# Decay attention, expert layer and gated convolution in one kernel: the start-up order of the constants, the zeros and the first loads

## The reference, cut to what matters

```python
# 1. attention with a per-head decay lam, no softmax; out per block of the sequence:
intra = (q @ k.T) * Dmask          # Dmask[i, j] = lam ** (i - j) where i >= j, else 0
out   = intra @ v + (q * lam ** (pos + 1)) @ kv_state
kv_state = lam ** block * kv_state + (k * lam ** (block - 1 - pos)).T @ v
# 2. mixture of 8 experts; each token goes to one expert e (its own argmax, or the token before's)
out = softmax(logits)[e] * (relu(x @ w1[e]) @ w2[e])
# 3. depthwise convolution of 5 taps, sigmoid, times x @ w_val, then @ w_out
```

## Time and profile before

| | |
|---|---|
| time, median of 3 runs | 390.23 us (389.72, 390.23, 396.63) |
| the profiled execution | 392.58 us, span from first to last instruction 390.7 us |
| PE busy | 374.4 us (96%) |
| DVE / ACT / POOL busy | 239.2 / 178.1 / 106.0 us |
| mean granted TensorE clock | 0.978 of full speed |
| DMA | 70.10 MB, 179 GB/s over the span |

### The profile page before, as it was taken

The page is one execution under the profiler, slowest core; times in us unless marked ns, Lnnn a source line. Parts: engine busy times, 40 slices in busy tenths (PEclk is TensorE's granted clock), DMA queues, the critical chain, the costliest instruction groups (busy, mean ns, idle before and its releaser), DMA issues.

```text
span 390.7 us, 6744 instructions
## 1 busy us (share of the span) xinstructions
PE 374.4 (96%) x2528; PEld 346.0 (89%) x2528; DVE 239.2 (61%) x488; ACT 178.1 (46%) x305; POOL 106.0 (27%) x98
## 2 busy tenths in 40 slices
PE   7999999999899999999999999999997989969987
PEld 7999999998898999989899898989996978959876
DVE  7656786687657192664728357283721799892930
ACT  1133354332126363645628355463711774937352
POOL 5325688484100000000000000000006865352640
PEclk9989999899999999999999999999999889998999
DMA  7999968341614739475692947645014601002012
GB/s 236 418 412 399 398 192 308 121 161 55 213 58 173 259 123 351 152 257 193 217 320 107 323 138 277 228 161 216 2 53 137 192 1 54 29 0 81 3 54 107
DMA packets 30761, 70.10 MB, mean 179 GB/s; under 512 B 2320, under 2 KB 2832, under 8 KB 30224
## 3 DMA queue, kind: packets, MB, share of 16 engines
q1 hardware_dynamic: 26192, 59.25, 42.4%
q0 software_dynamic: 1920, 6.29, 4.9%
q10 hardware_dynamic: 2624, 4.22, 2.9%
HBM read 55.08 MB, written 14.68 MB: 179 GB/s over the span
## 4 chain that ended last, share of the span: by engine, by line
PE 79%; DVE 12%; issue 3%; DMA 2%; ACT 2%; POOL 1%; DVEq 0%; POOLq 0%; ACTq 0%
PE bank L1161 75%; DVE gate L1109 5%; DVE w_raw L1109 3%; PE bank L1215 2%; PE bank L1316 2%; DVE x_all L1082 1%; DMA x_all<-y_slots,gather_u 1%; DMA lam_all<-lam 1%; DVE decay L846 1%; DMA y_slots<-y_out 1%; PE bank L1391 1%; POOL x_all L521 0%; ACT gate L751 0%; DVE w_sp L1074 0%; ACT w_sp L716 0%
## 5 line engine op out<-in xcount | busy, mean ns | idle before, releaser
L1161 PE MATMUL bank<-w_sp,h_sp 128*128 128x512 f32 (+1 forms) x480 | 106.4, 380 | 0.0
L1161 PEld LDWEIGHTS bank<-w_sp,h_sp 128*128 128x128 f32 x480 | 86.4, 188 | 16.3
L1161 PEld LDWEIGHTS bank<-x_sp,w_sp 128*128 128x128 f32 x768 | 93.2, 192 | 0.9 <-issue 0.3
L1161 PE MATMUL bank<-x_sp,w_sp 128*128 128x256 f32 x768 | 93.8, 283 | 0.1
L949 DVE TENSOR_TENSOR w_sp<-w_raw,w_sp 128x1024 fp32r<-128x1024 f32 x60 | 70.8, 1221 | 12.3 <-ACT w_sp L596 12.1
L596 ACT ACTIVATE w_sp<-w_raw 128x1024 fp32r<-128x1024 f32 x68 | 68.6, 1057 | 13.6 <-PE bank L1161 13.6
L521 POOL DMA_INDIRECT x_all<-y_slots,gather_u x12 | 12.4, 1030 | 193.0 <-DMA y_slots<-y_out 189.7
L1026 DVE SCALAR_TENSOR_TENSOR h_sp<-bank,h_sp 128x512 fp32r<-128x512 f32 x32 | 22.1, 689 | 63.6 <-ACT h_sp L636 62.6
L1161 PE MATMUL bank<-w_sp 128*128 128x384 f32 x192 | 39.1, 361 | 3.9 <-DVE prod L1124 1.7
L1161 PEld LDWEIGHTS bank<-w_sp 128*128 128x128 f32 x192 | 36.2, 204 | 6.1 <-DVE w_sp L1074 2.8
L636 ACT ACTIVATE h_sp<-bank 128x512 fp32r<-128x512 f32 x32 | 19.1, 598 | 48.1 <-PE bank L1161 48.1
(11 more groups left out here) (131 smaller groups left out, 443.5 us busy)
## 6 DMA issues: line engine op xcount, KB each, us to landing
w_raw<-w SPq DMA_DIRECT2D x32, 1024.0 KB, 5.8
qkv_sb<-qkv SPq DMA_DIRECT2D x22, 512.0 KB, 9.6
x_slots<-zeros SPq DMA_DIRECT2D x4, 1024.0 KB, 14.2
x_in<-x_slots SPq DMA_DIRECT2D x7, 512.0 KB, 6.6
y_slots<-y_out ACTq DMA_DIRECT2D x7, 512.0 KB, 5.3
out<-x_in SPq DMA_DIRECT2D x11, 256.0 KB, 2.0
w_raw<-w_val SPq DMA_DIRECT2D x1, 1024.0 KB
w_raw<-w_out SPq DMA_DIRECT2D x1, 1024.0 KB
```

What stands on the lines that cost most here:

```text
L1161: return nc.tensor.matmul(o, lhsT, rhs, start=start, stop=stop, skip_group_check=free)
```

## The change

SP issues tiles 2 and 3 straight behind tiles 0 and 1, then waits for `zeros_ok` alone, and then issues the four writes of zeros. POOL no longer clears `zeros`; DVE does, after its small tables and `hold`, and waits for that itself. DVE then waits for `lam_all` and runs the 8 decay scans and `k_decay`, which now releases `decay_ok`. The constants for the routing and `lam_pair` become `route_constants()`, called behind `mask(0)` and ahead of the `q_decay` scans. PE's first warm-up is 8 products, not 12.

```diff
@@ sync
             load_tile(0)
             load_tile(1)
+            load_tile(2)
+            load_tile(3)
             sp.wait_ge(zeros_ok, 1)
-            sp.wait_ge(warm_ok, 1)
             for n in range(SLOTS * DM // (P * UNIT)):
...
-                if n < 2:
-                    load_tile(2 + n)
@@ gpsimd
-            nc.gpsimd.memset(zeros[:, 2 * P:UNIT], 0.0).then_inc(zeros_ok, 1)
             pool.wait_ge(decay_ok, 1)
@@ vector
-            link(nc.vector.memset(no_add[:, :], 0.0))
+            nc.vector.memset(no_add[:, :], 0.0)
+            nc.vector.memset(hold[:, :, :], 0.0)
+            nc.vector.memset(zeros[:, 2 * P:UNIT], 0.0).then_inc(zeros_ok, 1)
+            dve.wait_ge(zeros_ok, 1)
             dve.wait_ge(lam_in, 16)
-            for s in range(2):
-                r = slice(s * D, (s + 1) * D)
-                last = nc.vector.tensor_copy(lam_pair[r, :], lam_all[r, :].rearrange("p (a s) -> p s a", s=2)[:, s, :])
-            link(last)
             dve.wait_ge(ident_ok, 2)
             for h in range(H):
...
-            dve.wait_ge(consts_ok, 5)
...
-            link(nc.vector.tensor_copy(k_decay[:, :, :], decay[:, :, :, P - 1:P].rearrange("p s a o -> p a (s o)")))
-            nc.vector.memset(hold[:, :, :], 0.0).then_inc(decay_ok, 1)
+            nc.vector.tensor_copy(k_decay[:, :, :],
+                                  decay[:, :, :, P - 1:P].rearrange("p s a o -> p a (s o)")).then_inc(decay_ok, 1)
+
+            def route_constants():
+
+                dve.wait_ge(consts_ok, 5)
...
+                for s in range(2):
+                    r = slice(s * D, (s + 1) * D)
+                    last = nc.vector.tensor_copy(lam_pair[r, :], lam_all[r, :].rearrange("p (a s) -> p s a", s=2)[:, s, :])
+                link(last)
...
                 mask(t)
                 if t == 0:
+                    route_constants()
@@ tensor
             pe.wait_ge(warm_ok, 1)
-            warm(12, ps_route)
+            warm(8, ps_route)
```

More of the change, by code:

```diff
@@ L848, in _ @@
             link(last)
-            dve.wait_ge(consts_ok, 5)
[L850 to L855, removed]
-            link(nc.vector.tensor_copy(k_decay[:, :, :], decay[:, :, :, P - 1:P].rearrange("p s a o -> p a (s o)")))
-            nc.vector.memset(hold[:, :, :], 0.0).then_inc(decay_ok, 1)
+            nc.vector.tensor_copy(k_decay[:, :, :],
+                                  decay[:, :, :, P - 1:P].rearrange("p s a o -> p a (s o)")).then_inc(decay_ok, 1)
+            def route_constants():
+                dve.wait_ge(consts_ok, 5)
+                nc.vector.tensor_copy(iota8_ps, iota8[:, :])
+                nc.vector.memset(ones_ps, 1.0)
+                nc.vector.memset(fresh_below[0:1, :], ALWAYS_FRESH)
+                nc.vector.tensor_copy(route_rhs[0:E, 0:E], ident[0:E, 0:E])
+                nc.vector.tensor_copy(route_rhs[0:E, E:E + 1], iota_col[:, :])
+                nc.vector.memset(route_rhs[Q:Q + E, E + 1:E + 2], 1.0)
+                for s in range(2):
+                    r = slice(s * D, (s + 1) * D)
+                    last = nc.vector.tensor_copy(lam_pair[r, :], lam_all[r, :].rearrange("p (a s) -> p s a", s=2)[:, s, :])
+                link(last)
             def mask(t):
```

## The result

The changed kernel takes 393.52 us (median of 14 runs), the kernel before 390.67 us in its 14 runs beside them. The ratio is 1.0079 with an interval of 1.0046 to 1.0111, so the change costs 3.1 us (1.8 to 4.3). That is less than the 2% that count here as a difference, and more than I forecast: 390.7 with a range up to 393.2, against 393.5. The changed start, as the traces show it, explains only part of the 3.1 us, so a second cause has to be found.

The account below looks back on a forecast made before the run. PE, busy 96% of the span, was taken as the bound, with time to save only at the start. From 390.23 us, -1.0 for the decay chain and +1.5 for the clock gave 390.7 us, range 388.0 to 393.2.

Parts of the forecast that it names:

- the sum: Whole kernel: -1.0 us for the decay chain, +1.5 for the clock, 0 for the rest, +0.5 in all.
- The behaviour behind 10 us is shifted as a whole: Everything after the start: moves with the start's change, with no further cost of its own.
- the clock's: PE at the start: the idle gap after the shorter warm-up brings a low clock over the scores, costing 1.5 us.
- one stretch of 3.4 us: PE from 6.6 to about 10 us: low clock over the scores, price taken as 1.6 us before deducting 0.1.
- the bound of 3.3: PE at the start: highest price of the low clock, 3.3 us, if it lasts until about 13.4 us.
- the likeliest case: Start: earlier decays gain 1.0 us, low clock over the scores costs 1.5; median 390.7 us, chance 0.47.
- rival (b): PE at the start: low clock outlasts the scores; if until 13.4 us, loss 2.3, 392.5 us; chance 0.10.
- rival (a): PE at the start: clock is high at the scores and stays high, only -1.0 stands, 389.2 us; chance 0.33.
- The clearing: DVE at the start: clearing the zeros takes 1.55 us, bounds 1.5 to 1.9, ending at 3.4 us.
- the gain: PE's keys_values(0): moves from 10.07 to 9.1 us through earlier decays, gain 1.0 us, bounds 0 and 1.1.
- Rival (c): Start: tile 0's second half lands near 8.8 us or decay_ok comes no earlier; say 391.2 us; chance 0.10.
- The constants: DVE behind mask(0): nine small routing instructions and lam_pair, 0.6 and about 0.4 us, cost 0 to 0.3, taken as 0.

Follow-up runs that it names:

- old_loads: The changed kernel with tiles 2 and 3 issued between the zero writes again, as before the change; ratio 1.0047 to the kernel before.
- again: The changed kernel itself, unaltered, run once more for a second profile; ratio 1.0079 to the kernel before.
- pad4: The changed kernel with 4 warm-up products more at the end of the attention stage, restoring PE's instruction count; ratio 1.0009 to the kernel before.
- warm4: The changed kernel with 4 products in the first warm-up instead of 8; ratio 1.0036 to the kernel before.
- late6: The changed kernel with 6 first warm-up products instead of 8, begun only when DVE has cleared the zeros; ratio 0.9992 to the kernel before, 0.9974 when repeated.
- late8: The changed kernel with its 8 warm-up products begun only when POOL has cleared the state; ratio 0.9980 to the kernel before.
- before_warm8: The kernel before with 8 first warm-up products instead of 12, nothing else; no ratio, six runs from 394.57 to 418.30 us.
- lam_act: The changed kernel with lam_all issued on ScalarE's queue, 11 first warm-up products and one more at the attention stage's end; ratio 0.9984 to the kernel before.

## Why the prediction was wrong

**The step that failed** is the last sentence of the sum: "The behaviour behind 10 us is shifted as a whole". A transfer 290 us later did not shift: it grew. The warm-up's four products were priced for the gap that they leave and not for their eight records of code. Their absence moved a 16 KB piece of program in among the data packets of the one write that all else waits for. That term was put at nothing; it measured 1.3 us up to the first gather in the shown pair of profiles, up to 1.7 in the others, 1.9 (to some 1.3) at the end of the spans, and 0.8 (to 1.4) by the timings. None of the rivals had it.

**A term of the right kind and too small** is the clock's. Forecast at 1.5, it is 1.8 in the traces and 2.4 (to 1.4) by the timings. The gap was 1.83 us (2.12 in the first profile; forecast 1.85), and a low stretch came in every trace with a gap. Its price can be added up from the same four groups of PE, against their full rate (1.68, 0.71, 1.13, 1.90). In the first profile of after it is 0.71 + 0.51 + 0.35 + 0 = 1.6; in old_loads 0 + 0.47 + 0.84 + 0.36 = 1.7: about the 1.6 taken for one stretch of 3.4 us, though it began later than thought. In `again` it is 1.38 + 0.51 + 0.78 + 0.12 = 2.8 and in pad4 3.2, nearly the bound of 3.3 that stood for a stretch to 13.4. On the first transposes these four are 0.33, 0.37, 1.59 and 1.84 later than in the kernel before, a mean of 1.0, where the forecast had a net 0.5. By price, the likeliest case and rival (b), in which the low clock outlasts the scores and which was given 0.10, came twice each (and (b) once more in warm4); in old_loads the scores themselves were fast, as rival (a) had it, and the low stretch came behind them. With 1.0 for the start and about 1.5 for the write the sum is 2.5, inside the measured 1.8 to 4.3.

**What held.** The clearing took 1.55 us; the scans ended at 6.45 (forecast 6.1; the clearing started 0.3 late); `k_scaled(0)` was then held by the second half of tile 0, at 8.11 (forecast 7.9, landing 8.0 rather than 7.8), so most of DVE's gain of 2.1 us was lost to that transfer, as said. With the clock left alone the gain was 0.8 (forecast 1.0). Rival (c) thus didn't come. POOL in fact did nothing while the 8 scans ran, and they took the 2.63 us of the earlier trace rows.

**What POOL beside the scans would have cost** is shown by the four scans of `q_decay`, which have two SBUF inputs as well. In the kernel before they took 2.15 us beside this:
```profile
10.50 1.23 POOL L463 TENSOR_TENSOR k_scaled<-qkv_sb,k_decay 128x512 f32<-128x512 f32 x1 [0.58 <-DMA qkv_sb<-qkv]
```
In the kernel after, with POOL idle by then:
```profile
12.24 1.37 DVE L961 TENSOR_TENSOR_SCAN q_decay<-lam_pair,no_add 128x128 f32<-128x128 f32 x4
```
In all traces it is 1.37 without POOL (five) and 2.15 to 2.25 beside `k_scaled` (eight). That agrees with the sharing that the Trainium skill describes, and the order of the change does well to keep POOL out of the way of the first scans.

**What cost nothing.** The zeros were issued from 5.7 us and the last landed at 7.3 + 19.6 = 26.9, ahead of the scatter. The second halves of tiles 2 and 3 landed 9.1 and 10.6 after their issues, by 15.6, and nobody was waiting. The constants, eight small instructions and not nine, took 1.7 us, from 10.49 to 12.2 (forecast 1.0), and delayed no one on the chain, which stays on PE.

**The range** ended at 393.2 because it reached to the dearest case of the start and to no further cause; the time lies 0.3 beyond. That it lies outside is partly chance: the forecast counted from 390.23, the median of three runs, and with 14 runs the kernel before has 390.67, 0.4 more. What is off without that chance is the size of the change, 3.1 (1.8 to 4.3) against 0.5.

**What stays open.** How the 3.1 us divide between the two causes in the timed runs is known only to about 1.4 us. Why PE is at the low level behind the gap for about 3 us in one execution and 6 in another isn't known, nor why the packet of program takes 1.0 us in one and 1.6 in another.

Lastly, late6 and late8 beat the changed kernel (0.9974 to 0.9992 against 1.0079; the intervals are apart, that of late6 by 0.0004 only), but not clearly the kernel before. What is left to win at the start, 0.7 us, is below what these timings tell.

## What to carry to other kernels

A warm-up belongs right in front of the work it is for. If it is shortened, shorten it at its beginning, by a wait in front of it, and leave no gap behind it: the same eight products ended in first transposes at 16.64 or at 14.30. When the number of instructions of an engine changes, read again the transfers that everything waits for, however far behind they are, for their landing and for an "instruction" queue among their packets; put the count back with work that waits anyway to see whether that is the cause. And when an engine is taken off the path, look for the transfer behind it first: of 2.1 us on DVE, 0.8 were there to be had.

## What the runs showed of the hardware

- Behind an idle gap of 1.6 to 2.1 us that followed 3.4 to 4.3 us of work, PE came to stand at its 1.2 GHz level in all six traces that have one (seven with warm4 and its 3.45 us). In `again`, pad4 and warm4 it was at the low rate already in the warm-up and stayed there to about 13 us. In the first profile of after, in old_loads, before_warm8 and lam_act it had risen, fell at 7.5 to 8.5, and stayed low for about 3 us in the first two and 14 in the others. In the kernel before, 1.10 us of idle time behind the scores cost nothing.
- The granted clock shows 1.00 ahead of its first record in a trace, whatever the rate. The number of records in a stretch is the safer reading: 17 and 18 against 32 in nearly equal lengths.
- Program code comes by DMA while the kernel runs, in 16 KB pieces. One piece among the packets of a 128 KB write made it land 3.3 to 3.9 us after issue instead of 1.7 with the piece behind it. The Trainium skill, DMA: Bandwidth & Descriptors, Queues, rings and completion order, has each DMA engine take turns between queues packet by packet. The traces agree: the piece's packet held one engine for 0.97 to 1.63 us, and the nine packets left, one engine's share, started when it was through.
- Four scans of VectorE with two SBUF inputs took 1.37 us alone and 2.15 to 2.25 beside an element-wise product on GpSimd (`k_scaled`).
- A 4 KB load issued on ScalarE's queue beside the 512 KB loads on SP's landed 6.3 us after its issue, and 2.6 when it was issued ahead of them on SP's.
